# Fourteen TensorE products on a zeroed tile ahead of the first attention scores

## The reference

```
scores = scale * matmul(q, k^T)                 # q, k, v: 4 x 8 heads x 576 x 64
thresh = max(scores) - tau
scores = where(scores >= thresh, scores, -1e9)
attn   = softmax(scores);  x = attn @ v         # 2304 tokens x 512
x      = gate * relu(x @ w1[e]) @ w2[e]         # e: the best of 8 experts of each token
h      = x @ w_in;  out = (h * tanh(softplus(h))) @ w_out
```

## Time and profile before

| | us |
|---|---|
| median of 3 runs | 940.85 |
| lowest and highest | 934.74 and 943.63 |
| the profiled execution | 939.59 |
| its span, first to last instruction | 938.0 |

### The profile page before, as it was taken

The page is one execution under the profiler, slowest core; times in us unless marked ns, Lnnn a source line. Parts: engine busy times, 40 slices in busy tenths (PEclk is TensorE's granted clock), DMA queues, the critical chain, the costliest instruction groups (busy, mean ns, idle before and its releaser), DMA issues.

```text
span 938.0 us, 19257 instructions
## 1 busy us (share of the span) xinstructions
PE 905.8 (97%) x7004; PEld 764.0 (81%) x7005; DVE 653.3 (70%) x1190; ACT 513.6 (55%) x1098; POOL 477.5 (51%) x557
## 2 busy tenths in 40 slices
PE   6999999999999999999889899999999999999997
PEld 4777777777778888888778788898889899889985
DVE  5898999989856111111233998888788788788793
ACT  4898888999871212121324655555455455555552
POOL 4222225556522490001300786786777777776885
PEclk9999999999999999999989899999999999999999
DMA  3122235433134940202081100001001000000000
GB/s 130 54 81 74 74 133 204 187 110 101 34 103 165 341 156 1 95 7 88 0 295 38 66 1 27 19 23 34 29 7 34 35 1 1 35 1 1 34 1 34
DMA packets 21448, 66.95 MB, mean 71 GB/s; under 512 B 3184, under 2 KB 3184, under 8 KB 20592
## 3 DMA queue, kind: packets, MB, share of 16 engines
q1 hardware_dynamic: 14432, 40.19, 12.9%
q0 software_dynamic: 4192, 20.00, 5.6%
q10 hardware_dynamic: 2736, 5.60, 1.9%
HBM read 47.22 MB, written 18.57 MB: 70 GB/s over the span
## 4 chain that ended last, share of the span: by engine, by line
PE 63%; DVE 4%; issue 2%; DMA 1%; ACT 1%; SPq 0%; POOL 0%; ACTq 0%; POOLq 0%; DVEq 0%
PE psum L1503 7%; PE psum L1504 6%; PE psum L1505 6%; PE psum L1493 6%; PE psum L1495 6%; PE psum L1494 6%; PE psum L1162 4%; PE psum L1163 4%; PE psum L1164 4%; PE psum L1177 4%; PE psum L1178 4%; PE psum L1176 4%; DVE rr L1632 2%; PE psum L1148 1%; PE psum L1477 1%
## 5 line engine op out<-in xcount | busy, mean ns | idle before, releaser
L1632 DVE RECIPROCAL rr<-rr 128x384 f32<-128x384 f32 x96 | 244.0, 2542 | 9.2 <-ACT rr L1569 9.2
L1246 DVE SCALAR_TENSOR_TENSOR hT_lo<-psum,hT_hi 128x512 fp32r<-128x512 f32 (+1 forms) x40 | 26.6, 664 | 157.2 <-ACT hT_hi L1223 157.0
L1493 PE MATMUL psum<-x2T_hi,w_in_hi 128*128 128x384 f32 x384 | 131.6, 343 | 1.1 <-DVE x2T_lo L1644 0.8
L1441 POOL TENSOR_TENSOR uu<-uu,ex 128x384 f32<-128x384 f32 x96 | 97.5, 1015 | 67.3 <-ACT uu L1561 67.2
L1495 PE MATMUL psum<-x2T_hi,w_in_lo 128*128 128x384 f32 x384 | 130.1, 339 | 0.0
L1494 PE MATMUL psum<-x2T_lo,w_in_hi 128*128 128x384 f32 x384 | 129.6, 337 | 0.0
L727 DVE TENSOR_SCALAR_CACHE_REDUCE ssb<-psum,tauk 128x576 f32<-128x576 f32 x144 | 112.6, 815 | 23.6 <-PE psum L426 20.4
L574 ACT ACTIVATE prob<-ssb,smin 128x576 f32<-128x576 f32 x144 | 113.0, 787 | 26.9 <-DVE ssb L727 26.2
L1503 PE MATMUL psum<-w_hi,g_hi 128*128 128x512 f32 x288 | 115.6, 401 | 2.6 <-DVE gg L1640 2.6
L1504 PE MATMUL psum<-w_lo,g_hi 128*128 128x512 f32 x288 | 115.1, 400 | 0.0
L1505 PE MATMUL psum<-w_hi,g_lo 128*128 128x512 f32 x288 | 115.0, 399 | 0.0
(11 more groups left out here) (215 smaller groups left out, 2070.4 us busy)
## 6 DMA issues: line engine op xcount, KB each, us to landing
qk<-in_qk_dram SPq DMA_DIRECT2D x15, 640.0 KB, 4.2
vsb<-in_v_dram SPq DMA_DIRECT2D x16, 512.0 KB, 3.7
xrow<-xs ACTq DMA_DIRECT2D x15, 288.0 KB, 3.2
ys<-ysb SPq DMA_DIRECT2D x4, 1028.0 KB, 5.8
wa<-in_wa_dram SPq DMA_DIRECT2D x8, 512.0 KB, 5.8
w_in_raw<-in_w_in_dram POOLq DMA_DIRECT2D x4, 1024.0 KB, 13.9
wb<-in_wb_dram SPq DMA_DIRECT2D x8, 512.0 KB, 14.0
yrow<-ys SPq DMA_DIRECT2D x4, 771.0 KB, 4.6
```

Source lines behind the costliest of these rows:

```text
L1493: pe.matmul(bank_of(n), w_in_hi[:, k, cols], xT_hi[w][:, k], start=(k == 0), stop=False)
L1632: dve.reciprocal(rr[:, n % 4], rr[:, n % 4]).then_inc(r_done, 1)
```

## The change

VectorE's stream now begins with a memset of the whole of `otsb` to zero, which signals a new semaphore, `idle_data`. TensorE's stream now begins with a wait for that semaphore and 14 float32 products: weights `otsb[:, 0, :]` (128 x 128), moving data `otsb[:, 1, 0:64]` (128 x 64), result in the first 64 columns of PSUM bank 0. That bank is written anew by `scores(0)`, which follows on the same engine and waits for nothing new. All other instructions and all transfers stay as they are.

```diff
+IDLE = 14
...
+    idle_data = sem("idle_data")
...
+        pe.wait_ge(idle_data, 1)
+        for _ in range(IDLE):
+            pe.matmul(psum[:, 0, 0:D], otsb[:, 0, :], otsb[:, 1, 0:D], start=True, stop=True)
         for c in range(NS):
             scores(c)
...
         factor, keep = tauk[:, 0:1], tauk[:, 1:2]
+        dve.memset(otsb[:], 0.0).then_inc(idle_data, 1)
         dve.wait_ge(tau_in, 16)
```

## The result

| | before | with the change |
|---|---|---|
| median of 20 runs | 938.97 us | 942.29 us |
| lowest and highest | 933.99 and 943.63 | 940.30 and 944.88 |
| profiled execution | 939.59 | 944.41 |
| its span | 938.0 | 942.8 |

The ratio is 1.0044, with a 95% interval of 1.0027 to 1.006, which is 2.5 to 5.6 us. The change is slower: 3.3 us between the medians, 4.8 between the two profiled executions. The time lies inside the stated range of 933 to 943 and inside the 1% that was called no change, but its sign is clear of noise, and the forecast of 2.65 us faster was wrong in sign.

The account below looks back on a forecast made before the run. TensorE, busy 97%, was taken as the bound. A 2.0 us block delay, then a faster clock, put scores(5) 2.65 us earlier: 936.9 from the profiled execution, 938.2 from the median, forecast 937.5 us, range 933 to 943.

Parts of the forecast that it names:

- What bounds the kernel, and the slow start: Whole kernel: TensorE bounds it, busy 97%; first products run at 1.2 GHz, later ones at 2.4; slow passes take 3.95 us.
- The memset: VectorE's start: costs VectorE nothing, as it idles until 4.61; takes about 0.31 us, so TensorE begins at about 1.3.
- The 14 products: TensorE's start: 28 records at 0.17 us end at 6.1, delaying scores(0) by 2.0 us; bounds for the end 4.3 and 8.3.
- the upper end: Upper bound for the block: 0.125 us a record at the fast rate, 0.25 at the slow; 28 take 7.0, end at 8.3.
- The rise at about 8: TensorE's start: unbroken work from 1.3 to about 10 us likely brings 2.4 GHz, placed at about 8, between 5 and 10.
- That it stays up: Passes after the rise: the fast clock holds, so passes take 3.04 us rather than 3.95.
- third rival: First passes: the rise comes and is lost in TensorE's gaps, or no net effect; 939 to 941 us, chance 0.1.
- The sum: First passes: scores(0) 2.0 us late, then faster passes; scores(5) at 20.5 against 23.17, 2.65 us earlier.
- pass 4: The pass from scores(4) to scores(5), TensorE's own: 5.29 us at the slow clock, 2.87 at the fast.
- The second: Rival 2, at the start: the block delays and brings no clock rise; slower, 941.6 up to 943.8 us, chance 0.2.
- So the 2.65 reach the end: After scores(5): TensorE bounds both kernels and later work hangs on earlier work, so the 2.65 us saved reach the end.

Follow-up runs that it names:

- half-width weights: The changed kernel with 64 instead of 128 weight columns in its 14 products: median 937.60 us against 937.61 before, ratio 1.0003.
- three wide products: The changed kernel with 3 products of 256 columns on zeros instead of 14 of 64: median 935.97 us against 937.93 before, ratio 0.9971.
- a wait, no products: The changed kernel without products, TensorE waiting for 20 memsets on VectorE instead: median 942.97 us against 937.93 before, ratio 1.0058.
- before, second look: The kernel before, unedited, profiled once more for its trace: that execution took 938.83 us.
- memset only: The changed kernel with the memset and TensorE's wait kept, no products: median 937.31 us against 938.81 before, ratio 0.999.
- seven wide products: The changed kernel with 7 products of 256 columns on zeros instead of 14 of 64: median 938.55 us against 937.93 before, ratio 1.0005.

## Why the prediction was wrong

Two steps failed: the price of a record of the block, and the fast clock that was to come at about 8 and stay.

- **What bounds the kernel, and the slow start:** right. The distances of 0.48 and 0.24 told the clock where the column had nothing recorded, and in every kernel that was fast early the passes fell from 3.95 to about 3.15 us.
- **The memset:** right. 0.27 us and TensorE's start at 1.41, for 0.31 and 1.3; alone it costs nothing that could be measured.
- **The 14 products: mis-sized, and the choice within the bounds was wrong.** I took 0.17 us a record from two weight loads that start 0.17 apart. They are the first two of a burst. In the change's block, too, the first two loads start 0.17 apart, but all later ones 0.21; with the longer ends it is 0.220 a record. The better row was the earlier trace rows, which I put down as the upper end: 0.125 at the fast clock, doubled. The delay is 3.5 us, not 2.0. The experiment with half the weight columns shows that their width is what sets it.
- **The rule of the page** (the Trainium skill, TensorE: Matmul & The Clock Gate, section on LDWEIGHTS: 107 ns for 128 columns) does not fit this block: with 128 weight columns in float32 and at 1.2 GHz a record takes 213 ns, twice the rule, and with 64 weight columns 107 ns, twice again. The trace decides against it there.
- **The rise at about 8: failed.** It came at 11.7, 11.5 and 10.1 in three traces (two of the change, one with nonzero data), each time during the score products and not in the block. The reason I gave, an unbroken stretch of eight or nine us, took every busy us for the same. In the blocks of wide products and of half-width weights, one trace each, it came at 4.5 to 5.7. What makes the difference was not isolated.
- **That it stays up: failed, and this cost the most.** I had it as a part of the third rival at 0.1. The clock fell at 15.1 in the first trace, at 14.9 and 13.6 in the others, each time after TensorE had idled 1.67 to 1.98 us ahead of `scores(2)`. But three wide products had 2.18 us of idling there and kept it, so the gap alone does not explain the fall; its cause stays open.
- **The sum.** `scores(5)` was expected at 20.5 and found at 25.81, 5.3 later. Step by step in the first trace: the block's end 1.5 (7.58 for 6.1); `scores(1)` still slow 0.4 (the copy of step 1 at 11.84 for 9.95, less the 1.5); the pass from step 2's copy to step 3's 0.9 (14.99 to 18.95, 3.96 for 3.04); pass 4 at the slow clock 2.4 (20.57 to 25.81, 5.24 for 2.87). So the block's price is 1.5 of the miss and the clock nearly all of the rest. Against the kernel before it was to be 2.65 earlier and was 2.64 later.
- **The rivals.** The second was the nearest: 941.6 to 943.8, measured 942.3. It said that all turns at pass 4, and that the change loses if the fast clock is not there when `scores(4)` starts; it started at 20.57 in a slow stretch. It was wrong in that the clock never rises. That it rises and is lost was the third rival, which put the time at 939 to 941. That the number fits the second so well is in part luck: it was counted from 939.59, and 20 runs put the kernel before at 938.97.
- **The baseline: an error that no step names.** The saving was counted from one trace in which the rise was at 22.8. Other executions of the same kernel have it at 8.3 or 13.3. Even three wide products, whose one trace has `scores(5)` 4.8 earlier than that one, moved the median by only 2.0 (by the ratio of 0.9971, 2.7).

"So the 2.65 reach the end" holds for the attention only. The table counts each trace against the first one of the kernel before, in us; a minus is earlier.

| trace | scores(5) | last scores of the attention | first product of the experts | span |
|---|---|---|---|---|
| the change | +2.6 | +2.9 | +5.6 | +4.8 |
| a wait, no products | +1.7 | +1.6 | +1.6 | +1.7 |
| before, second look | -3.1 | -2.7 | -0.6 | -0.8 |
| memset only | -3.0 | -3.6 | -2.7 | -2.7 |
| 3 wide products | -4.8 | -4.7 | -1.5 | -1.8 |
| half-width weights | -4.9 | -5.5 | -4.7 | -4.5 |

Until the last scores a shift is carried within 0.7 us, early or late, in all fourteen traces. At the border of attention and experts up to 3.1 us are lost. Five of the fourteen traces have a slow stretch there, between 271 and 282 us (both of the change, three and seven wide products, the second look at before), and TensorE's wait for a transfer ahead of it lasts 1.25 to 2.98 us. What decides either was not isolated.

## What to carry to other kernels

Work put into an idle engine's gap is free only until the data land; here a start 3.5 and 4.8 us late cost 3.3 and 5.0 us between medians. So size such a block by the steady pace of its records at the clock it will run at, not by the first two of a burst, and let it end early. Here the width of the weights, not the moving columns, set that pace. Before counting a saving against a trace, take the same kernel's trace a few times: what one execution shows at its start may be the worst of several.

## What the runs showed of the hardware

- A stream of float32 products with 128 x 128 weights and 64 moving columns runs at 0.213 us a record at 1.2 GHz (0.220 with its first and last), with 64 weight columns at 0.107 (0.113).
- A TensorE that reads as busy all the time (6.19 of 6.20 us) stayed at 1.2 GHz in three traces. In four traces with other products ahead of the scores (256 columns, or 64 with narrow weights) 2.4 GHz came at 4.5 to 5.7 us.
- Products on zeros can bring the rise: with seven wide ones it came at 5.4, before the first score product at 6.57. With 0.37 in place of 0 the narrow block looked the same, and the rise came after it as well.
- The clock can rise and fall again: up at 11.7, down at 15.1, up at 25.3 in the change. The first rise of an unchanged kernel lay at 8.3, 13.3 and 22.8 us.
